# Linear attention and two MLP layers in one kernel: GpSimd writes one item's diagonals, and the first group's work is put in another order

## The reference

```python
# _attn_ref: r, k, v are (4, 8, 768, 48), w and u (8, 48)
for t in range(S):
    kt, vt, rt = (k[:, :, t], v[:, :, t], r[:, :, t])
    cur = np.einsum('bhd,bhe->bhde', u[None] * kt, vt)
    y[:, :, t] = np.einsum('bhd,bhde->bhe', rt, state + cur)
    state = w[None, :, :, None] * state + np.einsum('bhd,bhe->bhde', kt, vt)
# reference: x is y as (3072, 384)
h = x @ w_in                                   # 384 -> 2048
x = (h * np.tanh(log1p(exp(h)))) @ w_out       # 2048 -> 384
h = x @ w_in2
out = np.where(h > 0, h, np.exp(np.minimum(h, 0)) - 1) @ w_out2
```

## Time and profile before

| | us |
|---|---|
| median of 3 runs | 872.03 (870.93 to 872.89) |
| the profiled execution | 871.44 |
| its span, first to last instruction | 869.6 |
| PE busy | 859.6 (99%) |
| DVE busy | 527.4 (61%) |
| ACT busy | 386.2 (44%) |
| POOL busy | 183.4 (21%) |

### The profile page before, as it was taken

One profiled execution on the slowest core, in us unless ns is written; L12 is line 12 of the kernel. 1 busy time (PEld: TensorE's weight loads), 2 busy tenths in 40 slices (PEclk: granted clock), 3 DMA queues, 4 the chain that ended last, 5 costly groups with the idle time before them and its releaser, 6 DMA issues.

```text
span 869.6 us, 14251 instructions
## 1 busy us (share of the span) xinstructions
PE 859.6 (99%) x6269; PEld 710.5 (82%) x6269; DVE 527.4 (61%) x518; ACT 386.2 (44%) x414; POOL 183.4 (21%) x112
## 2 busy tenths in 40 slices
PE   8999999999999999999999999999999999999998
PEld 7877788888888888888878888888888888888886
DVE  6699867777667777634458554454454454454443
ACT  6776766565667565666778320220220220220211
POOL 2663333354333353200245400000000000000000
PEclk9999999999999999999999999999999999999999
DMA  6553422212122221202223310010010000100100
GB/s 228 172 180 110 140 99 77 95 58 98 53 63 100 102 65 66 86 1 82 73 70 88 116 36 1 37 37 0 37 37 1 36 1 1 37 0 1 37 1 37
DMA packets 19056, 55.57 MB, mean 64 GB/s; under 512 B 2864, under 2 KB 4912, under 8 KB 18992
## 3 DMA queue, kind: packets, MB, share of 16 engines
q1 hardware_dynamic: 13968, 43.69, 14.9%
q10 hardware_dynamic: 5024, 10.95, 3.5%
HBM read 43.23 MB, written 9.44 MB: 61 GB/s over the span
## 4 chain that ended last, share of the span: by engine, by line
PE 91%; DVE 4%; ACT 3%; issue 2%; POOL 0%; DVEq 0%; ACTq 0%; POOLq 0%
PE y_ps L850 42%; PE h_ps L793 31%; PE a_ps L793 11%; PE a_ps L644 1%; PE a_ps L621 1%; PE a_ps L634 1%; DVE mid L1193 1%; PE h_ps L609 1%; DVE win_lo L1177 1%; DVE wout_lo L1177 1%; PE y_ps L651 1%; DVE g_hi L1184 0%; ACT mid L1031 0%; ACT mid L967 0%; DVE all_scores L1158 0%
## 5 line engine op out<-in xcount | busy, mean ns | idle before, releaser
L793 PE MATMUL h_ps<-x_split,win_hi 128*128 128x512 f32 (+1 forms) x864 | 265.9, 390 | 1.2 <-ACT mid L1032 1.2
L850 PE MATMUL y_ps<-g_hi,wout_hi 128*128 128x512 f32 x576 | 224.3, 389 | 2.4 <-DVE wout_lo L1177 1.3
L850 PE MATMUL y_ps<-g_lo,wout_hi 128*128 128x512 f32 x576 | 224.1, 389 | 0.0
L850 PE MATMUL y_ps<-g_hi,wout_lo 128*128 128x512 f32 x576 | 224.1, 389 | 0.0
L793 PEld LDWEIGHTS h_ps<-x_split,win_hi 128*128 128x128 f32 x864 | 159.6, 188 | 35.1 <-issue 1.4
L793 PE MATMUL h_ps<-x_split,win_lo 128*128 128x512 f32 (+1 forms) x432 | 166.8, 386 | 0.0
L1193 DVE TENSOR_TENSOR mid<-mid 128x1024 f32<-128x1024 f32 x48 | 77.5, 1615 | 109.4 <-ACT mid L967 109.4
L1186 DVE TENSOR_TENSOR g_lo<-mid,g_hi 128x1024 fp32r<-128x1024 f32 x96 | 134.1, 1397 | 3.3
L850 PEld LDWEIGHTS y_ps<-g_hi,wout_hi 128*128 128x128 f32 x576 | 108.1, 188 | 26.0 <-DVE g_lo L1186 2.7
L850 PEld LDWEIGHTS y_ps<-g_hi,wout_lo 128*128 128x128 f32 x576 | 108.1, 188 | 22.5
L850 PEld LDWEIGHTS y_ps<-g_lo,wout_hi 128*128 128x128 f32 x576 | 108.1, 188 | 22.4
(11 more groups left out here) (140 smaller groups left out, 844.7 us busy)
## 6 DMA issues: line engine op xcount, KB each, us to landing
att<-in_att SPq DMA_DIRECT2D x20, 584.0 KB, 5.4
att<-in_att SPq DMA_DIRECT2D x20, 512.0 KB, 3.7
w_raw<-in_w_in SPq DMA_DIRECT2D x16, 384.0 KB, 3.4
w_raw<-in_w_out SPq DMA_DIRECT2D x16, 384.0 KB, 3.0
x_dram<-mid ACTq DMA_DIRECT2D x6, 768.0 KB, 3.3
att<-x_dram SPq DMA_DIRECT2D x6, 768.0 KB, 4.5
out<-mid ACTq DMA_DIRECT2D x5, 768.0 KB, 3.9
mid<-in_first_T SPq DMA_DIRECT2D x2, 512.0 KB, 4.0
```

Of the source, the lines that this page charges most:

```text
L793: m = nc.tensor.matmul(ps, a, b_, start=n == 0, stop=n == len(terms) - 1)
L850: m = nc.tensor.matmul(y_ps[:, o, :], a, b_, start=unit == 0 and t == 0 and j == 0, stop=unit == UNITS - 1 and t == 1 and j == 2, skip_gro ...
```

## The change

Three things change, all in the first group.

- The diagonals of the last item (item 3) are no longer written by ACT's `first_fill`. POOL writes them with two `affine_select` instructions of 128x512 (`fill_last`), which keep the broadcast sums on the diagonal and write zero elsewhere. `mask_first(3)` waits for the new semaphore `last_diag`.
- ACT splits the first weight block ahead of the first own sums, where it stood behind item 0's diagonals.
- The order of the rest is new. ACT copies the second own sums between the two halves of item 0's diagonals, writes `k_wide` behind the high part of item 0, and splits the second weight block ahead of the high part of item 3. PE transposes `k_wide` behind the keys of item 2. DVE decays item 2 ahead of the low part of item 0.

What is left out at the top declares the semaphore `last_diag`.

```diff
@@ -472,6 +472,18 @@
                 k_, r_ = [kr_T(n)[:, i, :, :].rearrange("p a t -> p (a t)") for i in range(2)]
                 pool.tensor_tensor(kr_product[n % 2], k_, r_, ALU.mult).then_inc(product_done, 1)
 
+            def fill_last():
+
+                pool.wait_ge(own_done, PER)
+                pool.wait_ge(first_out_ps, 2)
+                sums = own[:, 1, :].rearrange("p (a s) -> p s a", s=2)
+                for hh in range(2):
+                    m = pool.affine_select(out=first_scores[1][:, hh, :, :],
+                                           in_=sums[:, hh, :].unsqueeze(2).to_broadcast([128, PAIRS, ITEM]),
+                                           compare_op=ALU.is_equal, fill=0.0, base=0, pattern=[[0, PAIRS], [-1, ITEM]],
+                                           channel_multiplier=1)
+                m.then_inc(last_diag, 1)
+
             pool.wait_ge(flag_done, 1)
             all_inside = pool.value_load(flag.bitcast(mybir.dt.int32))
 
@@ -568,6 +580,7 @@
                     pool.memset(token[:, 1:2], 0.0).then_inc(x_fixed, 2 * GROUPS)
                 first_product(2)
                 first_product(3)
+                fill_last()
                 pool.wait_ge(early_T, PER)
                 raw, hi, lo = w_views(0)
                 pool.wait_ge(w_hi_done, 1)
@@ -875,15 +888,15 @@
             first_main(0)
             first_own(2)
             first_states(0)
-            pe.wait_ge(k_wide_done, 1)
-            for p in range(PAIRS):
-                m = nc.tensor.transpose(y_ps[:, 1, p * ITEM:(p + 1) * ITEM], k_wide[:, p, :], ident)
-            m.then_inc(k_pow_ps, 1)
             first_main(1)
             first_own(3)
             first_states(1)
             first_item_scores(2)
             first_keys(2)
+            pe.wait_ge(k_wide_done, 1)
+            for p in range(PAIRS):
+                m = nc.tensor.transpose(y_ps[:, 1, p * ITEM:(p + 1) * ITEM], k_wide[:, p, :], ident)
+            m.then_inc(k_pow_ps, 1)
             first_item_scores(3)
             first_main(2)
             first_main(3)
@@ -991,30 +1004,28 @@
                 else:
                     act.dma_start(out[:, :, g * GROUP:(g + 1) * GROUP], y_sb).then_inc(out_stored, 16)
 
+            weight_hi(0)
             first_own(0)
             first_fill(0, 0)
+            first_own(1)
             first_fill(0, 1)
-            weight_hi(0)
-            first_own(1)
-            act.wait_ge(pow_done, 1)
-            act.activation(k_wide.rearrange("p a (b t) -> p a b t", t=C),
-                           pow_chunk[:, 0].unsqueeze(2).to_broadcast([128, PAIRS, 2, C]), ACT.Copy).then_inc(k_wide_done, 1)
             first_fill(1, 0)
             first_keys(0)
             first_fill(1, 1)
             first_keys(1)
             first_x_hi(0)
+            act.wait_ge(pow_done, 1)
+            act.activation(k_wide.rearrange("p a (b t) -> p a b t", t=C),
+                           pow_chunk[:, 0].unsqueeze(2).to_broadcast([128, PAIRS, 2, C]), ACT.Copy).then_inc(k_wide_done, 1)
             first_own(2)
             first_fill(2, 0)
             first_fill(2, 1)
             first_own(3)
             first_x_hi(1)
-            first_fill(3, 0)
-            first_fill(3, 1)
             first_keys(2)
             first_x_hi(2)
+            weight_hi(1)
             first_x_hi(3)
-            weight_hi(1)
             first_keys(3)
             act.wait_ge(k_pow_ps, 1)
             act.activation(k_pow, y_ps[:, 1, :].rearrange("p (h d) -> p h d", d=PAD)[:, :, 0:D], ACT.Copy)\
@@ -1119,7 +1130,10 @@
                 dve.tensor_tensor(t, t, pow_kr[:, :, :, :].rearrange("p i a t -> p (i a t)"), ALU.mult).then_inc(early_T, 1)
 
             def mask_first(n):
-                dve.wait_ge(first_diag, 2 * n + 2)
+                if n == PER - 1:
+                    dve.wait_ge(last_diag, 1)
+                else:
+                    dve.wait_ge(first_diag, 2 * n + 2)
                 dve.wait_ge(scores_ps, n + 1)
                 dve.copy_predicated(first_scores[n % 2].rearrange("p s a t -> p (s a) t"),
                                     later.bitcast(u32).unsqueeze(1).to_broadcast([128, H, ITEM]),
@@ -1215,11 +1229,11 @@
             dve.wait_ge(consts, 4)
             mask_first(0)
             mask_first(1)
+            decay_first(2)
             first_x_lo(0)
             dve.wait_ge(power_step, steps[0])
             dve.wait_ge(state_zeroed, 1)
             first_state_of(0)
-            decay_first(2)
             decay_first(3)
             first_x_lo(1)
             first_state_of(1)
```

More of the change, by code:

```diff
@@ L232, in attention_mlp @@
                                                      sem("w2_done"))
-        product_done, own_ps, own_done, first_diag = (sem("product_done"), sem("own_ps"), sem("own_done"),
-                                                      sem("first_diag"))
+        product_done, own_ps, own_done = sem("product_done"), sem("own_ps"), sem("own_done")
+        first_diag, last_diag = sem("first_diag"), sem("last_diag")
         first_k_ps, first_k_done, first_out_ps = sem("first_k_ps"), sem("first_k_done"), sem("first_out_ps")
```

## The result

The changed kernel takes 874.51 us (median of 7 runs, 872.63 to 875.99) against 872.47 us before (7 runs, 870.93 to 873.51): 1.0022 times as long, with a 95% interval of 1.0012 to 1.0032, or 1.0 to 2.8 us more. A second set of its runs, on the chip of the last experiments, gave 873.96 us and 1.0019 (1.0009 to 1.0029). The forecast was 875.0 us.

A forecast was written before the change was run, and what follows sets the result against it. PE was taken to bound the kernel, except from 33.7 to 68 us, where DVE does. 871.44 + 3.0 for late loads gave 874.4, as a median 875.0 us, range 871.6 to 877.6.

The forecast's parts named there:

- PE full before 33.7 us: First group: PE is busy 22.80 of 22.90 us, so only PE gains count; no new PE idle time there.
- The new order on ACT, -0.15 us: First group: PE's 0.15 us wait behind ACT's key copy goes, and no more than that.
- The sum: Whole program: 871.44 + 3.0 = 874.4 us, the 0.15 of PE lost waiting for POOL; as a median 875.0 us.
- GpSimd's diagonals, nothing: Item 3 on POOL: two selects, 1.2 us each, under a cover of 3.75 us; value 0, at most +1.0 us.
- Transposes, and the queue behind them: SP's third weight block waits for the later transposes; it and the loads behind it move by about 4.7 us.
- POOL and DVE by turns: 34 to 44 us: a shared SBUF port lock makes them wait; first tile's g at 43.9 us, +3.4; taken as +3.0.
- The loads of item 6, only 1.5 us late: Behind the first tile's g: these loads follow PE's work on item 4, some 1.5 us late.
- The first rival: Delay mostly absorbed as u lands earlier: median 873.4 us; sign, first tile's product before 42.3 us; chance 0.23 including no change.
- The faster rival: DVE's SBUF instructions slip past POOL's, two collisions avoided: 869.7 us, median 870.3; chance 0.07.
- the slow selects: GpSimd's selects at 2.4 us each hold up item 3's mask and PE: +1.0 on the forecast, 876.0 us; chance 0.06.

The follow-up runs named there:

- experiment two: The kernel before with only the four K-power transposes on PE moved behind the keys of item 2: 875.38 us, 1.0033.
- experiment six: The kernel before with only the change's new orders on ACT and DVE; transposes, GpSimd and loads as before: 871.87 us, 0.9996.
- experiment four: The changed kernel with spare products on PE ahead of item 4's main part: ten, 873.62 us, 1.0015; twelve, 873.89 us, 1.0011.
- experiment five: The kernel before with only item 3's diagonals written by GpSimd instead of ACT: 872.08 us, 0.9996.
- experiments one: The changed kernel with the K-power transposes put back ahead of item 1's output on PE: 871.73 us, 0.9996.
- Experiment three: The changed kernel with SP issuing the loads of items 4 and 5 ahead of the third weight block: 871.25 us, 0.9990.
- experiment seven: The changed kernel with u loaded from ACT's queue, behind the high part of item 2, instead of SP's: 874.05 us, 1.0016.

## Why the prediction was right

**PE full before 33.7 us.** Right: no new wait in any trace with the new PE order; the 0.75 us in experiment two is that of the old order on ACT.

**The new order on ACT, -0.15 us.** Mis-sized. It came from one execution in which the own sums were early. In the three other traces with the old order the wait was 0.75 to 0.78 us, and it is gone in all with the new one. The change thus gives back more than was counted; experiment two against the whole change says 0.9 us, 0.3 of it outside the span, experiment six 0.4, both within what the runs scatter. The sum also let the 0.15 us vanish in the wait for POOL. It does not: with the loads late, g starts 9.84 to 10.18 us behind the state of item 3 whether that state comes at 33.19 us (experiment four) or at 34.78 (experiment two), so what PE gains ahead of it is kept for the most part.

**GpSimd's diagonals, nothing.** Right. Each select took about 0.6 us, half of the assumed, and experiment five shows no change of the span. The 0.3 us around the span was no term of the forecast.

**Transposes, and the queue behind them.** Right, and the cause: experiments one, two and three switch the loss off, on, and off again. Experiment three brings the loads of items 4 and 5 and u forward together; which of them costs how much was not taken apart, beyond the half microsecond of u in experiment seven. The issue came at 22.86 us for 22.9. The load of item 4 was under-priced: expected at 27.2 us, POOL started at 29.04, since its load took 5.8 us to land and not 4.0. Three more loads were now issued within 1.5 us behind it; that it shared the rate with them is argued, not shown. u was used at 34.34 us for 33.3: its load took 8.7 us and landed at 34.2.

**POOL and DVE by turns.** The steps came out near: decay of item 5 to 39.66 us (39.5), diagonal copy to 40.25 (40.2), own sum at 42.20 (42.2), g at 43.62 (43.9). Single steps did not: DVE's third block went first, ahead of u, and its fourth waited for ACT, 1.34 us:

```profile
35.22 0.85 ACT L959 ACTIVATE win_hi<-w_raw 128x768 fp32r<-128x768 f32 x1 [3.53 <-DMA w_raw<-in_w_in]
```

ACT's split waited for the load of that block, until 35.2 us (34.8 forecast). By the end the steps are back within 0.3 us of the forecast's. The Trainium skill (SBUF — State Buffer, "SBUF: two separate sides") says of the port pair that DVE and GpSimd share that the instruction which starts first has it for its whole length. The row of 2.32 us agrees, and so does experiment seven, where an earlier product with u met DVE's third block, which ended at 35.03 us, and itself ended at 35.91, 0.88 us later, where a free-standing one takes 1.00.

**The loads of item 6, only 1.5 us late.** Wrong. They were issued at 44.69 us, where 41.69 was before, 3.0 us late: item 4's main part started 1.6 us later, and then, from its first product to that issue, took 3.6 us instead of 2.2 at the halved clock, which the forecast did not have. With the clock held up (experiment four) the loads came 1.4 us earlier, counted from the state of item 3, but by the 70th microsecond the trace was where it had been, 37.29 us behind that state for 37.31.

**The first rival**, that the delay is mostly absorbed, is excluded by its own sign: g started at 43.62 us, not before 42.3. What an earlier u would have done is shown only as far as experiment seven goes: it started POOL's product with u 0.5 us earlier, at 34.12 us, which is still behind the start of DVE's third block at 34.08, while the rival wanted POOL's next product done ahead of that block. The faster rival and the slow selects did not occur.

**The sum.** 871.44 + 3.0 = 874.4 against 874.51 in the profiled executions is close in part by luck: the execution of before was a fast one, by some 0.6 us of spare products and the wait behind them, and 0.5 us of the difference between the spans, 3.4 us, comes behind the stretch at 68 us, at one pause of PE at 179.6 us that the second trace of the changed kernel does not have. By the medians the loss is 2.0 and 1.7 us in the two sets, where the forecast put 3.0: the load queue costs what was forecast (3.0 in experiment two), and the terms that were too small are the gain on ACT (0.4 in experiment six, where the sum has nothing) and the time around the span (0.3 for nothing). Added up, 3.0 - 0.4 - 0.3 = 2.3 us. What stays open is how these share it out to the tenth.

## What to carry to other kernels

- A step on the compute side that releases a buffer can stand in front of a load queue. When it moves, count every load that is issued behind the one that waits, and put those that do not need the buffer ahead of it.
- Where two engines take turns, an earlier start of one step can be worth nothing by itself. Read the row of the instruction that is longer than its like, and see which instruction of the other engine ends with it.
- One profiled execution can hide a wait that most others have. Price an edit by the same place in several traces if there are any.

## What the runs showed of the hardware

- After 2.65 us without work PE's granted clock was at half, to past 44 us in one trace of the changed kernel and to past 47 us in the other. After 2.43 us (experiment two) it was too. It stayed at 1.00 after 0.85 us in the kernel before, and where ten spare products filled all but 0.46 us of the same gap.
- The seven 512-column products after the start took between 1.88 and 2.75 us in the traces, at a granted clock shown as 1.00 in all of them; later ones start 0.23 us apart. Their length decides where the first own sums start.
- A load of 192 KB on ACT's queue beside some 2.2 MB on SP's took 8.1 us to land, against 8.7 behind them on SP's, and 3.9 in the kernel before, issued 4 us behind the last of them.
- The time outside the span was 1.51 to 1.54 us in the kernels with GpSimd's selects and 1.83 to 1.85 in the four without, as means of their runs; experiment five against the kernel before has this difference with nothing else changed but the work that moved from ACT to GpSimd.
